# Attention and routed experts on one core: two DMA queues at the start, loads between bias steps, joint tile first, weights by runs into two raw buffers

## The reference

```
scores = q @ k.T / sqrt(64)
x = (log1p(|i-j|) / log1p(max(i,1)))          # 576 x 576
bias = relu(x * w1 + b1) @ w2                  # 32 hidden units, 8 heads
attn = softmax(scores + bias);  o = attn @ v   # -> x: 2304 tokens x 512
logits = x @ w_gate; gate = sigmoid(x @ w_local)
e[s] = argmax(logits[s]) if s == 0 or gate[s] < 0.5 else e[s-1]
out[s] = softmax(logits[s])[e] * (relu(x[s] @ W1[e]) @ W2[e])   # W1: 512x1024, W2: 1024x512
```

## Time and profile before

| | |
|---|---|
| median of 3 runs | 791.23 us (790.19 to 791.69) |
| the profiled execution | 790.51 us, of which the span is 788.8 us |
| PE busy | 665.3 us, 84% of the span |
| DVE, ACT, POOL busy | 386.6, 346.6, 206.4 us |
| bias phase | to about 81 us |
| attention | about 81 to 381 us |
| routing | about 381 to 433 us |
| experts | about 433 us to the end |

### The profile page before, as it was taken

The page is one execution under the profiler, slowest core; times in us unless marked ns, Lnnn a source line. Parts: engine busy times, 40 slices in busy tenths (PEclk is TensorE's granted clock), DMA queues, the critical chain, the costliest instruction groups (busy, mean ns, idle before and its releaser), DMA issues. The chain is left out here.

```text
span 788.8 us, 13394 instructions
## 1 busy us (share of the span) xinstructions
PE 665.3 (84%) x4323; PEld 530.1 (67%) x4323; DVE 386.6 (49%) x759; ACT 346.6 (44%) x707; POOL 206.4 (26%) x175
## 2 busy tenths in 40 slices
PE   2577799999999999999404799967599999999995
PEld 0122688888888888887204588855488788888883
DVE  2899466666556565556593342235542442222220
ACT  2599456566656666565310332224541442212221
POOL 2400334443444454440271011111121112111110
PEclk9799899999999999999755699998799999999999
DMA  4977414454434444440500421363331341111100
GB/s 95 205 195 194 106 29 97 110 108 108 95 91 102 96 91 94 101 92 17 216 12 28 172 85 51 146 231 138 127 124 40 133 152 40 50 43 40 40 13 0
DMA packets 68373, 77.03 MB, mean 98 GB/s; under 512 B 46959, under 2 KB 47471, under 8 KB 68336
## 3 DMA queue, kind: packets, MB, share of 16 engines
q1 hardware_dynamic: 64256, 65.02, 30.7%
q0 software_dynamic: 4080, 11.54, 4.4%
HBM read 144.56 MB, written 11.27 MB: 198 GB/s over the span
## 5 line engine op out<-in xcount | busy, mean ns | idle before, releaser
L689 DVE CUSTOM_DVE_ANT_0 sm<-ps_s,bias 128x576 f32<-128x576 f32 x128 | 91.9, 754 | 73.5 <-PE ps_s L931 66.9
L538 ACT ACTIVATE sm<-sm,negmax 128x576 f32<-128x576 f32 x144 | 111.9, 778 | 6.2 <-DVE negmax L689 6.2
L1079 PE MATMUL ps_s<-w1hi,xThi 128*128 128x512 f32 x200 | 67.7, 421 | 25.1 <-DVE w1lo L842 23.7
L868 DVE TENSOR_TENSOR hTlo<-ps_s,hThi 128x512 fp32r<-128x512 f32 x50 | 32.2, 686 | 104.7 <-ACT hThi L636 104.7
L1101 PE MATMUL ps_pv<-w2hi,hThi 128*128 128x512 f32 x200 | 80.5, 402 | 2.8 <-DVE w2lo L842 1.5
L1101 PE MATMUL ps_pv<-w2hi,hTlo 128*128 128x512 f32 x200 | 78.3, 391 | 0.0
L1101 PE MATMUL ps_pv<-w2lo,hThi 128*128 128x512 f32 x200 | 77.9, 390 | 0.0
L490 POOL DMA_INDIRECT out_dram<-ysb,sidx x25 | 25.3, 1010 | 192.1 <-ACT ysb L643 173.5
L1002 PE MATMUL ps_pv<-pT,vt 128*64 128x320 f32 (+1 forms) x512 | 69.1, 410 | 4.4 <-DVE pT L709 0.6
L438 POOL CAST ksplit<-raw 128x1152 fp32r<-128x1152 f32 x16 | 18.6, 1166 | 205.2 <-DMA raw<-in_kq_dram 143.5
L643 ACT ACTIVATE ysb<-ps_pv,pcur 128x512 f32<-128x512 f32 x25 | 17.2, 688 | 115.7 <-PE ps_pv L1101 105.4
(11 more groups left out here) (161 smaller groups left out, 1321.8 us busy)
## 6 DMA issues: line engine op xcount, KB each, us to landing
w1raw<-in_moe_w_dram SPq DMA_DIRECT2D x54, 1024.0 KB
w2raw<-in_moe_w_dram SPq DMA_DIRECT2D x54, 1024.0 KB
raw<-in_kq_dram SPq DMA_DIRECT2D x32, 432.0 KB, 4.9
bias<-stage SPq DMA_DIRECT2D x32, 288.0 KB, 3.2
raw<-in_kq_dram SPq DMA_DIRECT2D x32, 128.0 KB, 4.6
vt<-in_v_dram SPq DMA_DIRECT2D x32, 128.0 KB, 2.4
tokens_dram<-xl SPq DMA_DIRECT2D x64, 64.0 KB, 1.7
bias_tail<-stage SPq DMA_DIRECT2D x4, 144.0 KB, 2.4
```

Source lines behind the costliest of these rows:

```text
L538: nc.scalar.activation(probs, probs, ACT.Exp, scale=-1.0, bias=negmax[:, u % 2, hd:hd + 1], accum_out=sums[:, pr % 2, 2 * t + hd:2 * t + h ...
L689: nc.vector.tensor_tensor_reduce(sm[:, u % 2, S * hd:S * (hd + 1)].rearrange("p (a c) -> p a c", a=2), ps_s[:, hd, :, 0:HALF], bias.rearra ...
L868: V.tensor_tensor(hTlo[:, 4 * i:4 * i + 4, :].rearrange("p k t -> p (k t)"), ps_s[:, 1, i, :], hThi[:, 4 * i:4 * i + 4, :].bitcast(F32).re ...
L1079: last = nc.tensor.matmul(ps_s[:, 0, c, :], x[:, d, :], w[:, d, BANK * c:BANK * (c + 1)], start=d == 0 and x is xThi and w is w1hi, stop=d ...
```

## The change

Five things. (1) The first constants are started on two queues: SP starts the windows of groups 0 and 1, ACT those of groups 2 and 3 and the two small vectors; a group's four `rps` transfers are one. (2) Pair 0's q and k go out one DMA at a time behind bias steps 6, 9, ... 21, its v behind 28 and 29, the gate columns behind 31 and 32; pair 1's loads follow the last step. (3) Pair 0 is split on DVE, between its hidden units of step 33 and 34, not on POOL. (4) The joint tile's four steps come first, and DVE waits in pair 0 only for the bias rows of the tile at hand. (5) Expert weights have two raw buffers. A run is a row of tiles with one expert; SP loads run c+1 into buffer (c+1) mod 2 when the split of run c-1 is done, from a table per run. Experts 0 and 1 are loaded ahead. ACT and DVE read a tile's buffer number from a table into a register, and ACT also how many loads each buffer must have seen.

```diff
-            for pr in range(2):
-                load_qk(pr)
-                load_v(pr)
             for m in range(STEPS):
...
+                if 6 <= m < 6 + 3 * 2 * PARTS and m % 3 == 0:
+                    load_qk_part(0, (m - 6) // 3 // PARTS, (m - 6) // 3 % PARTS)
...
+            load_qk(1)
+            load_v(1)
...
+            for c in range(NE - 1):
+                b = (c + 1) % 2
+                e = nc.sync.value_load(run_i[0:1, 0, c:c + 1], min_val=0, max_val=NE - 1)
+                there = nc.sync.value_load(run_i[0:1, 1, c:c + 1], min_val=0, max_val=1)
+                split = nc.sync.value_load(run_i[0:1, 2, c:c + 1], min_val=0, max_val=NT) if c > 1 else 0
+                for i in range(2):
...
+                        sp.wait_ge(w1_lo, LEAD + split * 2 + i + 1)
+                    load_w1(b, i, e, {"cond": there})
...
@@ split_hi on ACT
                     act.wait_ge(used, LEAD + k)
+                    slot = nc.scalar.value_load(tile_i[0:1, 1, bass.ds(k, 1)], min_val=0, max_val=1)
+                    loads = [nc.scalar.value_load(tile_i[0:1, 2 + b, bass.ds(k, 1)], min_val=1, max_val=NE) for b in range(2)]
...
+                        for b in range(2):
+                            act.wait_ge(raw_in_s[b][i], loads[b] * 16)
+                        src = rawt[:, bass.ds(slot * (2 * n) + n * i, n), :]
...
@@ DVE
+                if m == STEPS - 3:
+                    split_first_pair()
             nc.vector.memset(ps_pv[D:P, 0:TAIL], 0.0).then_inc(corners, 1)
             nc.vector.memset(ps_pv[0:D, 2 * P + TAIL:2 * P + 2 * TAIL], 0.0).then_inc(corners, 1)
-            for i in range(SLOTS):
-                dve.wait_ge(bias_stored[i], stored(STEPS // SLOTS))
...
+                if pr == 0 and hd == 0:
+                    for i in range(SLOTS):
+                        dve.wait_ge(bias_stored[i], bias_rows_in(t))
```

More of the change, by code:

```diff
@@ L123, in build @@
     at[0] = SB0
-    w1raw, _ = place("w1raw", [P, KD, F], F32)
-    w2raw, _ = place("w2raw", [P, KF, DM], F32)
+    w1raw, _ = place("w1raw", [P, 2 * KD, F], F32)
+    w2raw, _ = place("w2raw", [P, 2 * KF, DM], F32)
     w1hi, _ = place("w1hi", [P, KD, F], F32R)
@@ L291, in _ @@
         def _(sp):
[L292 to L298, removed]
+            for g in range(2):
+                load_window(nc.sync, g)
             sp.wait_ge(zeroed, 1)
@@ L301, in _, with load_gates @@
                 nc.sync.dma_start(w2bd[C * g:C * (g + 1), H * g:H * (g + 1)], w2).then_inc(w2_in, 16)
-            sp.wait_ge(zeroed, 4)
-            for half in range(2):
+            def load_gates(half):
                 rows = slice(D * half, D * (half + 1))
@@ L312, in load_qk, with load_v_half, load_v @@
                 for half in range(2):
[L313 to L318, removed]
+                    for part in range(PARTS):
+                        load_qk_part(pr, half, part)
+            def load_v_half(pr, half):
                 s = pr % 2
                 vb = v[pr // PAIRS, :, P * (pr % PAIRS):P * (pr % PAIRS + 1)]
+                cols, k0, k1 = slice(D * half, D * (half + 1)), TAIL * half, P * FULL * (1 - half)
+                nc.sync.dma_start(vt[:, s, 0:FULL, cols],
+                                  vb[k0:k0 + P * FULL, cols].rearrange("(k p) c -> p k c", p=P)).then_inc(v_in[s], 16)
+                nc.sync.dma_start(vt[cols, s, FULL, cols], vb[k1:k1 + TAIL, cols]).then_inc(v_in[s], 16)
+            def load_v(pr):
                 if pr >= 2:
@@ L386, in _ @@
+            for b in range(2):
+                for i in range(2):
+                    sp.wait_ge(w1_in[b][i], 16 * (4 + b))
+                    sp.wait_ge(w2_in_e[b][i], 16 * (4 + b))
             sp.wait_ge(y_left, LEAD + NT)
@@ L512, in _ @@
                 act.sem_inc(x, LEAD)
+            nc.scalar.dma_start(w1s[:], w1c).then_inc(consts_in, 16)
+            nc.scalar.dma_start(b1s[:], b1c).then_inc(consts_in, 16)
+            for g in range(2, G):
+                load_window(nc.scalar, g)
             act.wait_ge(shift_made, 1)
@@ L703, in copy_a @@
                     dst = pT2[:, :, TAIL + P * (t - 2):TAIL + P * (t - 1)]
+                    if u == 2:
+                        for i in range(SLOTS):
+                            dve.wait_ge(bias_stored[i], stored(STEPS // SLOTS))
                     if t == 2 and pr:
```

182 lines of the change are left out of this document (128 added, 54 removed).

## The result

Measured side by side, the changed kernel takes 767.47 us (767.06 to 767.78, 4 runs) and the kernel before 791.46 (790.19 to 794.7, 4 runs): ratio 0.9695, 95% interval 0.967 to 0.9721. The profiled execution has a span of 766.0 us, 22.8 less than the 788.8 of before. PE's busy time fell by only 5.8 us (665.3 to 659.5), so most of what went is waiting.

The account below looks back on a forecast made before the run. PE bounds the last tiles; movable time lies in PE's waits at the start, in the bias phase and at the experts. From 790.5 us, -12.1 up to pair 1 and -11.1 in the experts give 767.3; 8-in-10 range 756 to 776.

Parts of the forecast that it names:

- start: First constants: fewer starts on two queues let DVE's `slope` begin at 6.9 us instead of 12.74; -5.8 us.
- bias steps and DVE's split: Bias phase: no loads or POOL split ahead, -8.8 us; DVE's own split of pair 0 in the open, +4.7.
- last step to first tile: From DVE's last hidden unit to the first attention tile: 4.2 us instead of 6.95; -2.7 us.
- attention: Pair 1: its loads start only after the last bias DMA, so PE waits for its split; +0.5 us.
- tile 1, both splits (tile 0 to 5): Experts, tile 1: ACT's register loads delay W1's split by 2.0 us, W2's by 1.0; +3.4 with slow matmuls.
- tile 5 to tile 10: Experts, new expert at tiles 6, 7 and 8: transfer waits go, splits remain, 10.8 us instead of 25.6; -14.8 us.
- tile 13 (tile 10 to 15): Experts, the last change of expert: grows by +0.3 us.
- Rival B: Bias phase held by its DMAs, loads behind steps and joint-tile starts; some 5 us, 772 us; chance 0.17.
- rival A: Experts: register loads hidden behind instructions already queued on ACT; 757 us; chance 0.15.
- C: Experts: each new 4 us wait drops PE to 1.2 GHz and eats the gain; 774.5 us; chance 0.12.
- D: Experts: transfers still come just in time, the 25.6 us stay and 3.7 come on top; 782 us; chance 0.05.
- E: Slower: after waits at tiles 1, 6 and 7 PE stays at 1.2 GHz for tiles; 803 at four; chance 0.03.

Follow-up runs that it names:

- one_queue: The changed kernel with all its 14 first transfers started on SP, none on ACT; 767.7 us, ratio 0.9716.
- loads_first: The changed kernel with pair 0's q, k and v loads started ahead of the bias steps instead of between them; 765.13 us, ratio 0.9679.
- split_pool: The changed kernel with pair 0's split back on POOL, run while the bias steps go on; 769.71 us, ratio 0.9735.
- no_runs: The changed kernel without expert weights by runs, loaded tile by tile into one raw buffer as before; 779.61 us, ratio 0.9864.
- packed: The changed kernel with one integer per tile, read once by ACT and DVE, register arithmetic replacing the loads in the splits; 757.79 us, ratio 0.9582.
- act_double: The changed kernel with each of ACT's three register loads in a split done twice; 787.04 us, ratio 0.9963.
- apart: The changed kernel with 22 first DMAs again, rps in four pieces a group, still on two queues; 768.37 us, ratio 0.9722.
- joint_last: The changed kernel with the joint tile's bias rows as the last four steps instead of the first four; 768.76 us, ratio 0.9724.
- only_runs: The kernel before with only the expert weights by runs, two raw buffers and their routing steps; 777.33 us, ratio 0.9828.

## Why the prediction was right

The time was 767 against 767.47, and the main terms were near theirs:

| term | predicted | measured |
|---|---|---|
| start | -5.8 | -5.1 |
| bias steps and DVE's split | -8.8+4.7 | -2.9 |
| last step to first tile | -2.7 | -2.5 |
| attention | +0.5 | +0.5 |
| routing | 0 | -0.2 |
| tile 1, both splits (tile 0 to 5) | +3.4 | +2.9 |
| tile 5 to tile 10 | -14.8 | -16.1 |
| tile 13 (tile 10 to 15) | +0.3 | +0.7 |
| sum | -23.2 | -22.8 |

That the sum is closer than its terms is luck: start and bias steps fell 0.7 and 1.2 us short, tile 1 and the stretch from tile 5 to 10 came out 0.5 and 1.3 better. Of the signs named beforehand four were missed: ACT did wait for a stage slot, the first tile came at 75.09 and not near 73, PE's wait for pair 1 was above 1 us, and those for `w2lo` were nearer 3 and 2 than 4. None of the three that would have proved the forecast wrong appeared: attention grew by no more than the 0.5 us forecast, ACT waits for no transfer in the loop, and tile 5 to tile 9 takes 57.7 us.

**Start.** Size right, reason half wrong. My working had 6.2 us by the starts on two queues and 6.4 by the transfers; the second held, and ended at 7.6. The landing of 2.2 us was also misread: it runs from the beginning of `b1s`'s start (10.52), and from the start's end it is 1.8. `one_queue` shows that the second queue adds nothing once 22 starts have become 14.

**Bias steps.** This step failed by 1.7 us: "Taken as 0, at most +3" for the slot. The cover of 2 us was worked out with a landing of 3.2, and the loads that share the engines raise it to 4.7; `loads_first` takes them away and both numbers go back. Rival B named the place and, at 5 us, overpriced it. The split's 4.24 for 4.7: a copy of 1152 columns took 0.76 us, where `hid`'s rate gave 1.0, and its start was covered by nothing, as said. `split_pool` confirms the trade.

**Last step to first tile, and pair 1.** 4.43 us for 4.2. From DVE's end to the end of POOL's split of pair 1 it is 20.3 us (70.66 to 90.93), forecast 20.2. The 0.9 us added for a slow PE behind DVE's split held. But I had not seen that the wait of 6.56 us had also cost PE its clock for pair 0's first tiles. With the clock back before them, PE wants pair 1 14.1 us after the first tile and not 15.7, so it waits 1.83 for 0.5 and is no later for it: the term came out right because two things that I had not seen cancel. That the clock is the cause rests on the windows above; no run changes it alone.

**Experts.** The mechanism held: no transfer is waited for in the loop, and what is left is the split with its register loads. Tile 1's wait rose by 2.16 where the term had 2.0, all of it on the path, and 1.64 go when arithmetic replaces the three loads. The waits at tiles 6, 7 and 8 were 2.99, 2.33 and 0.73 instead of 4.0, 3.9 and 0.8: where a cast to `hThi` still runs, ACT's stream already works on the register loads behind it (pieces of the chain of waits at the split of W2 for tile 6, then ACT's timeline there):

```profile
522.46 0.28 ACTq L657
522.74 0.18 ACT hThi L699
```

```profile
523.86 3.70 ACT L667 CAST w2hi<-w2raw 128x2048 fp32r x2 [0.75 <-issue]
```

ACT begins its copy 0.75 us after the casts, not 2.0; at the split of W2 for tile 1 it is 1.32. So rival A was partly true of these places and false of tile 1. At tile 13 I had priced W1's split alone; W2's adds a wait of 0.80 us, hence the row of tile 13 in the table.

**Rivals.** C came in small: the results behind tile 7's wait run slow (543.13 to 551.12), but from 515 to 575 us the clock is 0.97, not 0.83. D: the long waits are only in `no_runs`. E: no tile beyond the waits ran slow for its whole length. The Trainium skill ("DMA: Bandwidth & Descriptors", Latency and other measured facts) gives a register load a floor of about 600 ns. Here ACT's loads follow each other at 0.52 us (435.94 to 436.46), a little below that, and the measurement decides.

## What to carry to other kernels

A buffer that a register selects costs its engine the loads of those registers at the one moment when the buffer has just become free: pack what is needed into one integer, read it where the engine would wait anyway, and put no arithmetic behind the wait (on DVE 0.37 us from ACT's copy to its own operation with arithmetic, 0.15 with a load). Transfers placed into gaps of a busy store stream lengthen the stores' landing, so the cover of a ring of slots has to be counted with the longer landing. Fewer, larger first transfers were worth as much on one queue as on two. A wait that is removed may also give back the clock of the stretch behind it.

## What the runs showed of the hardware

- Register arithmetic is not free either: from `xThi` to the copy it is 0.04 us in the kernel before, 0.68 in `packed` with arithmetic, and 2.31 in the changed kernel with three loads.
- A DVE operation on `hid` beside one of POOL's split lasts about as long as POOL's: 2.86 us beside 2.69 in `split_pool`, instead of 0.57.
- When PE's clock rises differs from kernel to kernel with the same work at the same time. Windows of tile 0, whose first matmul stands at 425.49 in the changed kernel and at 425.78 in `act_double`, first of the one, then of the other:

```profile
429.00:432.00 3.00, 3.00 (x10) 2.31 (x9) 0.00 (x0) 0.00 (x0) 0.00 (x0) 0.60 1.03 403
```

```profile
429.00:432.00 3.00, 3.00 (x14) 2.43 (x13) 0.00 (x0) 0.00 (x0) 0.00 (x0) 0.94 1.02 401
```

With nearly the same wait (5.89 and 5.59 us) tile 0 to tile 1 took 16.18 us in the changed kernel and 14.92 in `apart`. The wait for tile 7's `w2lo` comes out in two sizes: about 2.3 us in the changed kernel, `joint_last` and `split_pool`, about 0.8 in `only_runs`, `one_queue`, `apart` and `loads_first`, where PE runs slow on the results of tile 6 already. These seven kernels have the same expert code, and their tiles 0 to 15 take 200.13 to 202.21 us. A microsecond more or less in this stretch is therefore no evidence for an edit by itself.
